# Moving the first MLP's weight loads to the GpSimd queue and reordering four engines around the attention work

## What is computed

```python
B, H, S, D = 4, 8, 576, 64            # attention, window of 64 keys, all float32
scores = q @ k.T / sqrt(D);  mask = (rel >= 0) & (rel < 64)
attn = softmax(where(mask, scores, -1e9));  x = attn @ v   # 2304 tokens x 512
# first MLP (d_ff 1536)
x = (sigmoid(x @ moe_w_gate) * (x @ moe_w_val)) @ moe_w_out
# second MLP (d_ff 1536)
return ((x @ moe2_w_a) * (x @ moe2_w_b)) @ moe2_w_out
```

## Time and profile before

| | |
|---|---|
| device time, median of 3 runs | 981.46 us (979.16 to 983.66) |
| the profiled execution, its own time | 979.16 us |
| its span | 977.4 us |
| PE busy | 946.1 us |
| DVE, ACT, POOL busy | 629.5, 479.9, 70.5 us |
| opening (to PE's first `fill` of chunk 0) | 0 to 40.3 us |
| first MLP with doubles 4 to 23 | 40.3 to about 533 us |

### The profile page before, as it was taken

How to read it: one execution, slowest core, us unless ns; L and a number is a source line. 1 busy time by engine, 2 the same in 40 slices (tenths; PEclk the granted TensorE clock), 3 DMA queues, 4 the chain that set the end, 5 groups by cost and what they waited for, 6 DMA issues and landing times.

```text
span 977.4 us, 16388 instructions
## 1 busy us (share of the span) xinstructions
PE 946.1 (97%) x5988; PEld 870.8 (89%) x5988; DVE 629.5 (64%) x1299; ACT 479.9 (49%) x943; POOL 70.5 (7%) x96
## 2 busy tenths in 40 slices
PE   5698899999999999999999999999999999999998
PEld 4698898888888888888899999999999999999998
DVE  4476677757667756764566657567666768654756
ACT  4676667665666556642334434434345425344233
POOL 1201201202111110210100000000010000010000
PEclk9699999999999999999999999999999999999999
DMA  7739868956986794774675488676687766777672
GB/s 169 196 106 269 258 185 244 294 147 207 262 243 191 213 264 136 249 225 139 212 256 186 151 307 307 238 265 250 237 323 261 266 248 239 265 278 274 220 255 107
DMA packets 208143, 223.38 MB, mean 229 GB/s; under 512 B 84928, under 2 KB 165824, under 8 KB 205760
## 3 DMA queue, kind: packets, MB, share of 16 engines
q1 hardware_dynamic: 207104, 219.19, 69.5%
q0 software_dynamic: 960, 3.15, 0.8%
HBM read 179.83 MB, written 42.47 MB: 227 GB/s over the span
## 4 chain that ended last, share of the span: by engine, by line
PE 85%; DMA 5%; DVE 3%; SPq 3%; ACT 2%; issue 1%; DVEq 0%; ACTq 0%
PE ps L594 13%; PE ps L712 13%; PE ps L713 13%; PE ps L714 13%; PE ps L596 13%; PE ps L595 13%; DMA w_raw<-in_moe_w_out 3%; PE ps L586 2%; PE ps L561 2%; PE ps L574 1%; DMA out<-ost 1%; SPq L440 1%; DVE p_out L1127 1%; PE ps L547 1%; PE ps L544 1%
## 5 line engine op out<-in xcount | busy, mean ns | idle before, releaser
L594 PE MATMUL ps<-x_hi,gv_hi 128*128 128x512 f32 (+1 forms) x480 | 181.6, 378 | 0.1
L596 PE MATMUL ps<-x_hi,gv_lo 128*128 128x512 f32 (+1 forms) x480 | 177.4, 370 | 0.0
L595 PE MATMUL ps<-x_lo,gv_hi 128*128 128x512 f32 (+1 forms) x480 | 177.2, 369 | 0.0
L712 PE MATMUL ps<-xc,wc 128*128 128x384 f32 x504 | 171.3, 340 | 0.0
L714 PE MATMUL ps<-xc,wc 128*128 128x384 f32 x504 | 170.3, 338 | 0.0
L713 PE MATMUL ps<-xc,wc 128*128 128x384 f32 x504 | 170.2, 338 | 0.0
L1205 DVE TENSOR_TENSOR tt<-ps,tt 128x384 f32<-128x384 f32 x108 | 59.3, 556 | 86.2 <-PE ps L714 85.8
L594 PEld LDWEIGHTS ps<-x_hi,gv_hi 128*128 128x128 f32 x480 | 90.9, 189 | 12.6 <-issue 1.1
L596 PEld LDWEIGHTS ps<-x_hi,gv_lo 128*128 128x128 f32 x480 | 90.7, 189 | 11.6
L595 PEld LDWEIGHTS ps<-x_lo,gv_hi 128*128 128x128 f32 x480 | 90.9, 189 | 10.5
L1087 DVE TENSOR_TENSOR gv_lo<-w_raw,gv_hi 128x1024 fp32r<-128x1024 f32 x59 | 73.2, 1240 | 41.0 <-ACT gv_hi L824 41.0
(11 more groups left out here) (104 smaller groups left out, 1504.0 us busy)
## 6 DMA issues: line engine op xcount, KB each, us to landing
wc<-wprep SPq DMA_DIRECT2D x54, 1024.0 KB, 6.9
wc<-wprep SPq DMA_DIRECT2D x54, 768.0 KB, 5.7
wprep<-p_out SPq DMA_DIRECT2D x18, 1792.0 KB, 7.1
w_raw<-in_moe_w_gate SPq DMA_DIRECT2D x60, 256.0 KB, 3.6
w_raw<-in_moe_w_val SPq DMA_DIRECT2D x60, 256.0 KB, 3.9
w_raw<-in_moe_w_out SPq DMA_DIRECT2D x60, 256.0 KB, 4.7
v_nat<-in_v SPq DMA_DIRECT2D x64, 128.0 KB, 4.3
k_nat<-in_k SPq DMA_DIRECT2D x40, 128.0 KB, 3.0
```

The source lines that it names most:

```text
L594: pe.matmul(dst, w_h, m_h, start=first, stop=False)
L595: pe.matmul(dst, w_h, m_l, start=False, stop=False)
L596: return pe.matmul(dst, w_l, m_h, start=False, stop=last)
L712: pe.matmul(dst, w_h, m_h, start=k in (0, 1, 3) and t == 0, stop=False, skip_group_check=True)
```

## The change

Weight loads of the first MLP go from SP to POOL: the first two at once, the third behind `filled` 3, then `w_ring` for each step with `weight_sums` of a unit behind it. SP's opening order closes the gaps (v of double 1 ahead of q and k of double 3). In the opening PE does `mix` ahead of the next `score`, ACT does `mix_hi` ahead of the `exps` after it and the `split_first` quarters earlier, and DVE does both halves of a `normalise` together and `mix_lo` ahead of them. In the steps of the chunks DVE does `normalise` behind `split_gv` and `unfill`, `hidden` ahead of `mask_and_max` (except at f = 0), and `weights_lo` ahead of `hidden`.

```diff
@@ pool
+            def w_ring(c, f):
+                s = c * STEPS + f
+                for ready in (gv_hi_ready, gv_lo_ready, wo_hi_ready, wo_lo_ready):
+                    pool.wait_ge(ready, s - W_SLOTS + 1)
+                weight_dmas(pool, f)
...
-            for t in range(PREP_UNITS):
-                weight_sums(t)
+            for f in range(W_SLOTS):
+                if f == 2:
+                    pool.wait_ge(filled, 3)
+                weight_dmas(pool, f)
+            for s in range(W_SLOTS, CHUNKS * STEPS):
+                w_ring(s // STEPS, s % STEPS)
+                if prep_at(s - W_SLOTS) is not None:
+                    weight_sums(prep_at(s - W_SLOTS))
@@ sp
             load_qk(sp, 2)
+            load_v(sp, 1)
             load_qk(sp, 3)
-            load_v(sp, 1)
-            weight_dmas(sp, 0)
+            load_v(sp, 2)
             load_qk(sp, 4)
-            load_v(sp, 2)
-            weight_dmas(sp, 1)
             load_v(sp, 3)
             load_qk(sp, 5)
-            sp.wait_ge(filled, 4)
-            weight_dmas(sp, 2)
...
-                if s + W_SLOTS < CHUNKS * STEPS:
-                    w_ring(s + W_SLOTS)
@@ tensor, opening
             fill(first[3])
-            score(first[2])
             mix(first[0])
+            score(first[2])
             turn(first[1])
+            mix(first[1])
             score(first[3])
-            mix(first[1])
@@ scalar, opening
             copy_k(first[3])
+            mix_hi(first[0])
             exps(first[2], 0)
-            mix_hi(first[0])
             turned_copy(first[1])
             exps(first[2], 1)
+            split_first(0)
+            mix_hi(first[1])
             exps(first[3], 0)
-            mix_hi(first[1])
...
@@ vector, a chunk's step
-                    if to_turn:
-                        normalise(to_turn, 0, 2)
-                        to_mix = to_turn
                     if f + 1 < STEPS or c < CHUNKS - 1:
                         split_gv(c, f + 1)
                     if d and f > 0:
                         unfill(d)
+                    if to_turn:
+                        normalise(to_turn, 0, 2)
+                        to_mix = to_turn
                     split_wo(s, f)
-                    if d:
+                    if d and f == 0:
                         mask_and_max(d, 0)
                         mask_and_max(d, 1)
-                    hidden(s, f, w)
                     if prep_at(s - 1) is not None:
                         weights_lo(prep_at(s - 1))
+                    hidden(s, f, w)
+                    if d and f > 0:
+                        mask_and_max(d, 0)
+                        mask_and_max(d, 1)
@@ vector, opening
             normalise(first[0], 0, 1)
+            normalise(first[0], 1, 1)
             mask_and_max(first[1], 0)
-            normalise(first[0], 1, 1)
             mask_and_max(first[1], 1)
             unfill(first[3])
+            mix_lo(first[0])
             normalise(first[1], 0, 1)
+            normalise(first[1], 1, 1)
             mask_and_max(first[2], 0)
-            mix_lo(first[0])
-            normalise(first[1], 1, 1)
             mask_and_max(first[2], 1)
...
```

More of the change, by code:

```diff
@@ L425, in store_x2 @@
                              staged[:, :, 0:w]).then_inc(stored, 16)
[L427 to L431, removed]
             def load_weights(t):
@@ L1017, in _ @@
             copy_k(first[3])
+            mix_hi(first[0])
             exps(first[2], 0)
-            mix_hi(first[0])
             turned_copy(first[1])
             exps(first[2], 1)
+            split_first(0)
+            mix_hi(first[1])
             exps(first[3], 0)
-            mix_hi(first[1])
             turned_copy(first[2])
             exps(first[3], 1)
-            split_first(0)
+            split_first(1)
             mix_hi(first[2])
-            split_first(1)
+            split_first(2)
             turned_copy(first[3])
-            split_first(2)
             split_first(3)
@@ L1346, in _ @@
             normalise(first[0], 0, 1)
+            normalise(first[0], 1, 1)
             mask_and_max(first[1], 0)
-            normalise(first[0], 1, 1)
             mask_and_max(first[1], 1)
             unfill(first[3])
+            mix_lo(first[0])
             normalise(first[1], 0, 1)
+            normalise(first[1], 1, 1)
             mask_and_max(first[2], 0)
-            mix_lo(first[0])
-            normalise(first[1], 1, 1)
             mask_and_max(first[2], 1)
+            mix_lo(first[1])
+            split_first(0)
             normalise(first[2], 0, 1)
+            normalise(first[2], 1, 1)
             mask_and_max(first[3], 0)
-            mix_lo(first[1])
-            normalise(first[2], 1, 1)
             mask_and_max(first[3], 1)
+            split_first(1)
+            mix_lo(first[2])
             normalise(first[3], 0, 1)
-            split_first(0)
-            mix_lo(first[2])
             normalise(first[3], 1, 1)
-            split_first(1)
             split_first(2)
```

## The result

The changed kernel takes 1013.49 us (median of 4 runs, 1012.67 to 1014.82), the kernel before 980.79 us (4 runs, 979.16 to 983.66). The ratio is 1.0332, with a 95% interval of 1.0304 to 1.0359: slower by 33 us, where 986 (977 to 996) was forecast. The profiled executions have spans of 1012.4 and 977.4 us, 35.0 apart.

A forecast was written before the change was run, and what follows sets the result against it. PE was taken as the bound, busy 946.1 of 977.4 us, so only some 31 us could be won. 979.16 - 7.8 + 7.8 + 1.8 + 2.4 + 1.5 = 984.9, carried to 986.0 us for the median; range 977 to 996.

The forecast's parts named there:

- Part 1, late weights, -7.8: Chunk 0: weight loads on POOL wait only for their slot, removing PE's two waits for `turned_copy`, -7.8 us.
- The 0 for POOL's issue: POOL: three DMAs cost 1.7 to 5.0 us to issue, sums still end in time for `weights_hi`; taken as 0.
- the rival in which POOL is late: POOL: three DMAs take over 6.3 us to issue, sums come late and PE waits at `mix`; 996 us, chance 0.12.
- Part 2, chunk 0, +7.8: Chunk 0: DVE's order delays `normalise`; `turn` waits 1.4 us in five doubles and 0.8 in one, +7.8 us.
- Part 2, later chunks, +1.8 (0 to 6): Later chunks: POOL's sums stretch `hidden` or gv_lo in nine doubles, 0.2 us each, +1.8 us, bounds 0 to 6.
- The slack of 0.3 us: Later chunks: `normalise` ends 0.3 us before PE wants `turn`; no wait if nothing on DVE is stretched.
- `weights_lo` ahead of `hidden`, 0: DVE in the chunks' steps: this order costs nothing, since `down` wants the hidden values one step later.
- Part 3, +2.4: Opening orders: cycles from `turn` to `turn` of 7.55 and 7.3 us instead of 5.8, +2.4 us (1 to 3.5).
- The half of 2.3 us: Whole kernel: half the gap from fastest to median execution carried for late weights, taking 984.9 to 986.0 us.
- Part 4, +1.5 (0 to 3.5): Opening: the first two weight loads run beside q, k and v and delay k, +1.5 us (0 to 3.5).
- 0 at the chunk ends: The end of a chunk had no waits to win and was given no cost of its own.
- the opening +3.9: Opening: +2.4 us for the new orders and +1.5 us for the early weight loads, taken together.

The follow-up runs named there:

- e7: The kernel before with only the weight loads from step 3 on moved to POOL, sums behind them, first three loads left on SP: 972.78 us, ratio 0.9909.
- e4: The changed kernel with POOL's four sums of a unit each replaced by a memset of the same output: 992.13 us.
- e10: The changed kernel with `weights_lo` alone put back behind `hidden`: 1011.36 us, ratio to before 1.0308.
- e3: The kernel before with the new opening orders of PE, ACT and DVE alone, loads as before: 981.80 us, ratio 1.0013.
- e1: The changed kernel with DVE's order in the chunks' steps as before; POOL loads and new opening orders stay: 978.61 us, ratio to before 0.9979.
- e6: The kernel before with only the POOL and SP hunks, first two weight loads at once; PE, ACT and DVE orders as before: 978.53 us, ratio 0.9979.
- e2: The kernel before with DVE's new order in the chunks' steps alone, loads still on SP: 992.67 us, ratio 1.0125.
- e5: The changed kernel with all three first weight loads waiting for `filled` 3, behind the `fill` of double 2: 1008.31 us.
- e12: e6 with all three first weight loads, on POOL, waiting behind the `fill` of double 2: 972.53 us, ratio to before 0.9912.
- e9: The changed kernel with the masking alone put back ahead of `hidden`; gv_lo stays ahead of `normalise`: 986.14 us, ratio to before 1.0056.

## Why the prediction was right and wrong

**Part 1, late weights, -7.8: right.** The chunk 0 pairs of e7 add up to 80.7 us against 88.1, that is -7.4, and the whole comes to -9.3 (by the two profiled executions 979.16 and 973.15, -6.0, for before had an unusually quick opening there, see part 3). The 0 for POOL's issue held: three DMAs take 0.76 + 0.75 + 0.55 = 2.06 us, near the lower bound of 1.7, and the rival in which POOL is late did not occur. The transfers were not the limit in chunk 0; the order on SP was.

**Part 2, chunk 0, +7.8: right by its own working, and not enough.** Waits of 1.46 and 0.49 us stand where 1.4 and 0.8 were worked out. With 17.0 and four times 17.8 the chunk would take what it took before, and e4 shows just that (88.2 us). What was missed is the other two pairs, 22.73 + 21.61 - 2 x 17.8 = 8.7 us, a collision term that the working put at nothing in chunk 0: `h_lo` held for 2.88 us, a wait of 3.78, and behind it the lower clock. The windows show it (columns as in the earlier trace rows; the granted clock is the seventh value), 0.50 (1.2 GHz) behind the long wait, where it was 1.00 behind one of 1.46:

```profile
80.00:84.00 4.00, 3.65 (x42) 3.41 (x42) 3.37 (x4) 2.20 (x2) 2.05 (x3) 1.00 0.20 53
...
100.00:104.00 4.00, 3.62 (x14) 3.63 (x15) 3.37 (x4) 2.32 (x2) 2.06 (x3) 0.50 0.25 50
```

**Part 2, later chunks, +1.8 (0 to 6): the step that failed, +16.3.** The slack of 0.3 us and the place of the collisions were seen; the size was not. I took one stretched instruction of the earlier trace rows, 0.55 us, as the price of a collision and let 0.2 of it through. In fact `h_hi` and `h_lo` are both hit in the ordinary step, 1.29 + 1.11 where e4 needs 0.48 + 0.69: 1.23 us later. Less the slack of 0.3 that is 0.93, and the pairs are 1.06 longer. Where the subtraction is caught at the first of the sums it loses 2.98 - 0.69 = 2.3 us, the length of three sums. That length, 3 x 0.75 us, against a slack of 0.3, should have been the bound for each of the nine doubles that lie in a preparation step: up to 1.95 us each, 17.6 in all, where collisions cost 11.9 by e4. The other 4.4 us are the order's own: 2.4 of them at the end of chunk 0, where the last double's `turn` waits 1.15 us (the prediction counts that double in chunk 0, at 1.4) and `down` 0.99. (PE was not busy in every stretch from 120 us on, as the prediction reads it: behind 409.17 us it was idle for 5.5 of 568.23 us before, but that stretch grew by only 0.8.)

**`weights_lo` ahead of `hidden`, 0: wrong at four places.** The argument that `down` comes a step later fails at the last step of a chunk, where `down` follows at once: waits of 0.75 to 0.99 us, 3.3 in all, and e10 measures 2.1 us for them.

**Part 3, +2.4: the cycle right, its price not.** e3's timeline has `turn`s 7.5 and 7.2 us apart, as worked out (7.55 and 7.3), though the first two `turn`s came at 16.01 and 23.00, not at 15.4 and 22.5:

```profile
30.51 0.33 PE L574 MATMUL ps<-ident,probs_a 128*128 128x128 f32 x1 [1.77 <-DVE probs_a L1067]
...
37.69 0.48 PE L574 MATMUL ps<-ident,probs_b 128*128 128x128 f32 x1 [2.92 <-DVE probs_b L1067]
```

But e3's ratio is 1.0013, 1.3 us, and e1 against e6 shows 0.1. In e2 and e7, whose openings are the old ones, the first `fill` of chunk 0 stands at 42.53 and 42.79, not at 40.27 as in the earlier trace rows; in e3 it stands at 43.02. The profiled execution of before was the quickest of its runs, and its opening was not typical; a difference against it overstates what orders cost. What makes the old opening vary by 2 us was not settled. The half of 2.3 us that the prediction carried for late weights, as what varies between executions, was a guess: no run takes it apart, though the six runs of e7 lie within 1.2 us and the eleven of before beside them within 5.5.

**Part 4, +1.5 (0 to 3.5): too small, 5.2 (e5) to 6.0 (e6 to e12).** Both streams were taken to share and the q and k loads to be mostly done. The wait of 5.41 us for k shows they were not, and by DVE's order the whole of it went down the chain.

**The sum by its terms:** -7.8 and +7.8 stand; +1.8 should have been +16.3, and another +8.7 in chunk 0; 0 at the chunk ends some 2 (within the 16.3); the opening +3.9 was +8.8 against this profile, of which some 5.8 are the early loads (49.03 against 43.16 in e5) and 1.5 the orders (49.03 against 47.58 in e6). So the range failed because its upper end for collisions was taken from the one collision that the trace showed, not from the longest that the new order allows.

## What to carry to other kernels

A move of loads to another queue is worth what it takes out of an order, and should be tried by itself: here it wins 0.9% (e7), and what came with it costs 4% on top of e7. Before operations are put ahead of a hand-over with 0.3 us of slack, ask which of them another engine can hold up, and for how long at the most; put those behind the hand-over (e9). A bulk load that is wanted later should not start beside small ones on which the opening waits.

## What the runs showed of the hardware

A DVE subtraction with both inputs in SBUF was not let in between back-to-back sums of POOL: `h_lo`, 0.69 us by itself, took 2.98, from 0.30 us before the first sum to 0.48 us behind the start of the fourth, the only one with a pause of 0.07 us ahead of it. The cast `h_hi`, with one input, is held as well: 1.29 us beside sums where it takes 0.48 beside memsets. It is also longer beside some of POOL's DMA issues (0.73 us at 260.74 in e4), while `h_lo` keeps its 0.69 there. And issuing from POOL cost 0.76 us for 512 runs of 512 B and 0.55 us for 128 runs of 2 KB: four times the runs took 1.4 times as long:

```profile
L231 POOL DMA_DIRECT2D w_raw<-in_moe_w_gate x60 | 45.6, 760 | 389.9 <-DVE wo_lo L1102 379.2 <-PE ps L548 10.8
...
L233 POOL DMA_DIRECT2D w_raw<-in_moe_w_out x60 | 33.0, 550 | 0.0
```
